# Attention and two feed-forward layers on one core: w_out's rounding copies move to ScalarE, layer 2's weight mixing to GpSimd, and two pieces of work change their place in their engine's order

## The reference, cut to what matters

```python
scores = scale * np.matmul(q, k.transpose(0, 1, 3, 2))
scores = np.where(block_i >= block_j, scores, -1000000000.0)
attn = np.exp(scores - np.max(scores, axis=-1, keepdims=True))
x = (attn / (np.sum(attn, axis=-1, keepdims=True) + 1e-09)) @ v      # heads side by side: (2304, 512)
h = x @ w_in;   g = h * np.clip(h + 3.0, 0.0, 6.0) / 6.0;  x = g @ w_out     # layer 1
h = x @ w_in2;  g = h * np.tanh(log1p(exp(h)));            y = g @ w_out2    # layer 2
```

## Time and profile before

| | us |
|---|---|
| median of 3 runs | 978.65 (973.37 to 980.71) |
| profiled execution | 975.95 |
| its span | 974.0 |
| PE busy in it | 952.0 (98%) |
| DVE, ACT, POOL busy | 746.6, 643.6, 431.3 |
| granted clock, mean | 0.998 |

### The profile page before, as it was taken

How to read it: one execution, slowest core, us unless ns; L and a number is a source line. 1 busy time by engine, 2 the same in 40 slices (tenths; PEclk the granted TensorE clock), 3 DMA queues, 4 the chain that set the end, 5 groups by cost and what they waited for, 6 DMA issues and landing times.

```text
span 974.0 us, 17754 instructions
## 1 busy us (share of the span) xinstructions
PE 952.0 (98%) x6028; PEld 848.0 (87%) x6028; DVE 746.6 (77%) x1417; ACT 643.6 (66%) x1431; POOL 431.3 (44%) x410
## 2 busy tenths in 40 slices
PE   8999999999999999999899999999999999999998
PEld 7898888999887888888788988998998988988896
DVE  7898898774868686789788787777887777777654
ACT  7999999754544445454445557777777777776663
POOL 7899779665837596776867670000000000000000
PEclk9999999999999999999999999999999999999999
DMA  7988898657698978788786546555655654565255
GB/s 217 270 240 243 258 273 234 173 153 238 220 291 291 290 256 252 234 294 252 269 275 212 209 170 217 176 202 195 215 197 184 231 210 155 182 248 187 90 193 194
DMA packets 84601, 216.42 MB, mean 222 GB/s; under 512 B 10144, under 2 KB 16928, under 8 KB 84512
## 3 DMA queue, kind: packets, MB, share of 16 engines
q1 hardware_dynamic: 84368, 215.01, 67.6%
q10 hardware_dynamic: 144, 0.29, 0.1%
HBM read 162.07 MB, written 39.92 MB: 207 GB/s over the span
## 4 chain that ended last, share of the span: by engine, by line
PE 67%; DVE 7%; DMA 6%; SPq 4%; POOL 3%; issue 2%; ACT 1%; ACTq 0%; DVEq 0%; POOLq 0%
PE psum L1021 32%; PE psum L904 10%; PE psum L906 10%; PE psum L905 10%; DMA ext_d<-ext_made 3%; PE psum L849 2%; PE psum L828 2%; DVE ebuf L1624 1%; PE psum L808 1%; POOL osplit L1885 1%; SPq L646 1%; DVE glo L1630 1%; PE psum L809 1%; SPq L648 1%; DVE ext_made L1530 1%
## 5 line engine op out<-in xcount | busy, mean ns | idle before, releaser
L1021 PE MATMUL psum<-ghi,osplit 128*128 128x512 f32 (+1 forms) x640 | 216.7, 372 | 2.1 <-POOL osplit L1885 2.1
L904 PE MATMUL psum<-xhi,whi 128*128 128x256 f32 (+1 forms) x640 | 188.0, 294 | 5.1 <-ACT snap L1242 2.5
L906 PE MATMUL psum<-xhi,wlo 128*128 128x256 f32 (+1 forms) x640 | 187.2, 293 | 0.0
L905 PE MATMUL psum<-xlo,whi 128*128 128x256 f32 (+1 forms) x640 | 187.0, 292 | 0.0
L1021 PE MATMUL psum<-osplit,ghi 128*128 128x512 f32 x576 | 180.7, 395 | 1.3 <-DVE glo L1630 1.3
L1630 DVE SCALAR_TENSOR_TENSOR glo<-ebuf,ghi 128x512 fp32r<-128x512 f32 x144 | 126.5, 878 | 22.9 <-ACT ghi L1290 14.8
L904 PEld LDWEIGHTS psum<-xhi,whi 128*128 128x128 f32 x640 | 121.1, 189 | 19.0 <-ACT snap L1242 4.4
L1290 ACT ACTIVATE ghi<-ebuf 128x512 fp32r<-128x512 f32 x144 | 90.4, 628 | 66.9 <-DVE ebuf L1624 46.2
L1021 PEld LDWEIGHTS psum<-ghi,osplit 128*128 128x128 f32 x640 | 118.5, 190 | 18.4 <-issue 2.7
L1885 POOL TENSOR_TENSOR osplit<-oraw,osplit 128x512 fp32r<-128x512 f32 x80 | 117.2, 1468 | 38.1 <-ACT osplit L1209 34.0
L905 PEld LDWEIGHTS psum<-xlo,whi 128*128 128x128 f32 x640 | 121.2, 189 | 10.5
(11 more groups left out here) (120 smaller groups left out, 2147.4 us busy)
## 6 DMA issues: line engine op xcount, KB each, us to landing
ext<-ext_d SPq DMA_DIRECT2D x56, 768.0 KB, 4.4
osplit<-o_d SPq DMA_DIRECT2D x80, 512.0 KB, 5.3
oraw<-in_w_out SPq DMA_DIRECT2D x80, 256.0 KB, 5.8
wraw<-in_w_in SPq DMA_DIRECT2D x26, 512.0 KB, 6.0
ext_d<-ext_made SPq DMA_DIRECT2D x32, 384.0 KB, 6.2
attn_t<-ostage SPq DMA_DIRECT2D x32, 288.0 KB, 3.7
qkin<-in_qk SPq DMA_DIRECT2D x30, 288.0 KB, 3.7
kparts<-kparts SPq DMA_DIRECT2D x30, 288.0 KB, 4.2
```

The source lines that it names most:

```text
L904: pe.matmul(dst, hi, xh, start=(start and cc == 0), stop=False, skip_group_check=True)
L905: pe.matmul(dst, hi, xl, start=False, stop=False, skip_group_check=True)
L906: last = pe.matmul(dst, lo, xh, start=False, stop=(stop and cc == 1), skip_group_check=True)
L1021: last = pe.matmul(bank(Y_BANK + c, n), stat, mov, start=(first and m == 0), stop=(final and m == 2), skip_group_check=True)
```

## The change

Four edits, all in layer 1's steps:

1. The high halves of w_out's tiles 32 to 79 are made by ACT (split_o_hi in relu_period) and no longer by POOL.
2. The three subtractions of layer 2's extra jobs (steps 19 to 26) are made by POOL (mix_late, with the new semaphore late_mixed), after the step's first low half of w_out, and no longer by DVE.
3. On DVE, extra_jobs and ahead_os of a layer 1 step stand behind the step's two relu products and the first low half of g, no longer before them.
4. On POOL, in step 0, mix_x(1, 1) stands behind the low half of the step's second w_out tile.

```diff
-ACT_OS = TILE0[FIRST_STEP[2]]
 SPLIT_OS = TILE0[LAYER]
...
-MIXED = [sum(3 if e else 1 for _, _, _, e in JOBS[NEARLY:m]) for m in range(len(JOBS) + 1)]
+MIXED = [sum(0 if layer == 1 and e else 3 if e else 1 for layer, _, _, e in JOBS[NEARLY:m])
+         for m in range(len(JOBS) + 1)]
...
             def split_ext_hi(m):
                 layer, p, _, _ = JOBS[m]
-                act.wait_ge(w_mixed, MIXED[m + 1])
+                if layer == 0:
+                    act.wait_ge(w_mixed, MIXED[m + 1])
+                else:
+                    act.wait_ge(late_mixed, 3 * (p + 1))
...
             def first_os(s, k):
 
-                todo = [i for i in splits_at(s) if i < ACT_OS]
+                todo = [i for i in splits_at(s) if i < SPLIT_OS]
...
             def mixing_jobs(s):
                 for m in jobs_at(s)[0:1]:
-                    mix_w(m)
+                    if JOBS[m][0] == 0 or JOBS[m][2]:
+                        mix_w(m)
...
-                extra_jobs(s - 1)
-                ahead_os(s - 1)
                 relu6_times_h(s + 1, 0)
                 relu6_times_h(s + 1, 1)
                 split_g_lo(s + 1, 0)
+                extra_jobs(s - 1)
+                ahead_os(s - 1)
                 mixing_jobs(s)
...
+            def mix_late(m):
+
+                p, raw = JOBS[m][1], wraw[m % 2]
+                a11, a12, a22, a21 = (raw[:, k * A_COLS:(k + 1) * A_COLS] for k in range(4))
+                pool.wait_ge(w_loaded[m % 2], w_level(m))
+                nc.gpsimd.tensor_tensor(a21, a11, a21, ALU.subtract).then_inc(late_mixed, 1)
+                pool.wait_ge(late_mixed, 3 * p + 1)
+                nc.gpsimd.tensor_tensor(a22, a22, a21, ALU.subtract).then_inc(late_mixed, 1)
+                pool.wait_ge(late_mixed, 3 * p + 2)
+                nc.gpsimd.tensor_tensor(a12, a12, a22, ALU.subtract).then_inc(late_mixed, 1)
...
             def split_o(i):
                 o, raw = osplit[i % OS2], oraw[i % OR]
-                if i < FIRST_OS or i >= ACT_OS:
+                if i < FIRST_OS:
...
                 if s == 0:
                     add_x(1, 3)
                     scale_x(1, 3)
-                    mix_x(1, 1)
+                for m in jobs_at(s):
+                    if JOBS[m][0] == 1 and JOBS[m][3]:
+                        mix_late(m)
                 next_x(s, 0)
                 for i in todo[1:2]:
                     split_o(i)
+                if s == 0:
+                    mix_x(1, 1)
                 next_x(s, 1)
```

More of the change, by code:

```diff
@@ L368, in build @@
         w_mixed = sem("w_mixed")
+        late_mixed = sem("late_mixed")
         w_hi = sem("w_hi")
@@ L1881, in split_o @@
                     nc.gpsimd.tensor_copy(o[:, 0:D], raw[:, :]).then_inc(o_hi, 1)
-                    pool.wait_ge(o_hi, i + 1 if i < FIRST_OS else i + 1 - (ACT_OS - FIRST_OS))
+                    pool.wait_ge(o_hi, i + 1)
                 else:
```

## The result

The changed kernel takes 981.23 us (median of 17 runs, 979.46 to 985.83), the kernel before in the same rounds 975.7 (17 runs, 972.48 to 981.07): ratio 1.0068, 95% interval 1.0054 to 1.0082. That is inside the forecast range, but on the other side of the forecast: about 6 us slower, not 1 us faster. The profiled execution took 979.46 us, its span 977.4 us against 974.0; granted clock 0.998 in both.

What follows compares the result with a forecast made beforehand. PE was taken as full from 600 us, with about 14 us reachable in its earlier waits and slow clock. Terms -1.1 - 1.7 - 1.4 - 0.3 - 1.0 + 2.8 + 1.7 = -1.0 us: 975.95 to 975.0, range 963 to 985.

Steps and rivals of the forecast that it cites:

- DVE's order: Moving extra_jobs and ahead_os later on DVE: -1.4 and -0.3 us of PE waits, +3.2 us on block 4's x load.
- The -1.4 at step 10: PE's 1.46 us wait at 317.56 for DVE's relu product, behind the jobs, would go: -1.4 us.
- Steps 0 and 1: Moving mix_x(1, 1) behind a split gains 1.1 us net; the half clock after the wait goes, another 1.7 us.
- Step 17: POOL's chain for block 3 loses five casts, so PE's 1.04 us wait at 401.80 goes: -1.0 us.
- Step 12: PE's wait at 341.98 for ACT's copy goes with DVE's new order: -0.3 us.
- Block 4's chain: x loads and POOL work needed by step 26 take 93.6 us from step 18 against 90.8: PE starts later by 2.8.
- the first rival: POOL is fast enough in steps 18 to 26, nearly all waits go: -11 us, 965 us; chance 0.22.
- The clock: PE's wait of 3 to 4 us before step 26 brings the half clock: +1.7 us.
- The ring (2): Moved DVE job, w_out's loads and ACT hold each other up, 18 us at 7.5 us landing: 988 us; chance 0.10.
- the sign that the prediction named for it: From step 11 on PE would wait for ACT while ACT waits for oraw.

Runs made afterwards that it cites:

- edit 1 with mixing in four steps: Kernel before, with w_out's high halves (tiles 32 to 79) on ACT and POOL mixing layer 2 only in steps 19, 22, 23, 26: ratio 0.9976.
- the jobs between the products: extra_jobs and ahead_os put between DVE's first and second relu product, in several kernels; against the changed kernel's ratio 1.0068, the changed kernel with this: 0.9982.

## Why the prediction was wrong

**The step that failed** is "DVE's order". It saw that SP's queue waits for the moved job and priced the later x load for block 4 only. That price was right: x went out 5.4 us into step 18 (5.6 forecast).

```profile
406.60 0.61 SPq L647 DMA_DIRECT2D xst<-attn_t  x1
```

But the same queue carries block 2's x and w_out's tiles in steps 3 to 10, and there the chain had almost no cover either: before, its last split ended 42.6 us after step 6's start, at 314.29, and PE's first matmul on it came 0.2 us later, without a wait; now the split ends after 45.5.

```profile
314.52 0.29 PE L904 MATMUL psum<-xhi,whi 128*128 128x256 f32 x1
```

Step 9 grew by 2.84 us, 2.58 of it the wait for this split, and the sum had nothing for it; of the changes that were not forecast it is the largest. The place of the jobs behind the second product was read from the order of the list. When that product can run in the new order was not followed (in step 8 it waits 6.63 us, in part for a store in the very queue that the job holds up), although the prediction's own rows for step 18 showed the job 3.5 us late. The -1.4 at step 10 failed too: DVE came 1.30 us late again (1.46 before), 12.13 us for the step. This step varies between executions of the same work: edit 1 alone and edit 1 with mixing in four steps are one program up to step 19 and took 12.49 and 10.89 us; with the jobs between the products it was 10.57 in three kernels and 12.17 in a fourth.

**Steps 0 and 1.** They gained 1.67 us of the 2.8 forecast (1.1 and 1.7), and not by edit 4. In the kernel with edit 1 alone, whose program is the same as before up to step 11, they take 25.1 us. The row answering to the first of the earlier trace rows:

```profile
213.16 0.36 PE L1020 MATMUL psum<-ghi,osplit 128*128 128x256 f32 x1 [1.16 <-POOL osplit L1884]
```

Its wait is 1.16 us, not 2.10, and the clock stays 1.00. Of the twelve profiled kernels without edit 4 (before included) ten take 24.7 to 25.5 us there and two 27.4; the seven with it take 25.1 to 26.1. So before's profile showed an unlucky execution, and I took its 2.10 us and its half clock for the kernel's own; edit 4 alone measures 1.0003. The forecast had no wait left for tile 4 and one of 1.0 us for tile 5. Measured are 1.03 for tile 4, whose low half POOL could start only at 209.39, when ACT's high half was there, and which took 1.80 us, and 0.37 for tile 5: the sum of the two is near, the places are not.

**Step 17**: -1.34 (1.0 forecast), right. **Step 12**: -0.56 (0.3), right.

**Block 4's chain**: right in sum, 94.59 from step 18 to 26 (94.3 forecast: 2.8 on 91.55), and by the places named: ACT held by POOL's mixes in steps 21 and 25 (waits of 1.40 and 0.8), the x split before step 26. Its parts were not right, so that the sum came out is luck. SP's weights load in step 22, then the rows that answer to the earlier trace rows:

```profile
451.06 0.33 SPq L586 DMA_DIRECT2D wraw<-in_w_in  x1
...
417.70 1.30 POOL L1851 TENSOR_TENSOR xst<-xst 128x512 f32<-128x512 f32 x1 [0.65 <-DMA xst<-r_d]
...
445.33 3.18 POOL L1888 TENSOR_TENSOR xlo<-xst,xhi 128x512 fp32r<-128x512 f32 x2
...
464.91 1.29 POOL L1851 TENSOR_TENSOR xst<-xst 128x512 f32<-128x512 f32 x1 [3.55 <-DMA xst<-r_d]
...
491.26 3.11 POOL L1888 TENSOR_TENSOR xlo<-xst,xhi 128x512 fp32r<-128x512 f32 x2
```

What ended last runs through the load of the second half. It went out at 453.00, 51.8 us after step 18's start, 47.5 before: in step 22 too SP stood for the moved job (its weights load comes 6.2 us into the step, 1.2 before), and the forecast had charged that to step 18 alone. From the issue to the first add it took 11.9 us, 14.5 before, which I had not counted; from there to the last split 29.5, 27.4 before. That is 4.4 - 2.6 + 2.0 = 3.8 us later, where 4.2 was forecast.

First add to last split took 30.8 and 29.5 us in the two halves, before 28.3 and 27.4: 4.6 more, where my terms gave about 2. The four mixes cost 13.2 us (10.8 forecast), the two waits for ACT's high half 3.0 (2.2), the ten casts that left gave back 10.0 (8.9), and the other operations, the same in both kernels, took 1.6 us less: the lighter contention on POOL came, at 1.6 of the 2.2 forecast. The groups between 401 and 496, then two groups of the kernel before (400 to 494) that go with the earlier trace rows:

```profile
L1829 POOL TENSOR_TENSOR wraw<-wraw 128x256 f32<-128x256 f32 x7 | 8.8, 1264 | 0.0
L1831 POOL TENSOR_TENSOR wraw<-wraw 128x256 f32<-128x256 f32 x7 | 8.4, 1194 | 0.6
L1833 POOL TENSOR_TENSOR wraw<-wraw 128x256 f32<-128x256 f32 x7 | 5.2, 739 | 0.5
L1635 DVE SCALAR_TENSOR_TENSOR glo<-ebuf,ghi 128x512 fp32r<-128x512 f32 x17 | 21.1, 1239 | 7.7 <-ACT ghi L1294 7.5
L1534 DVE TENSOR_TENSOR ext_made<-wraw,ext_made 128x768 fp32r<-128x768 f32 x7 | 12.1, 1727 | 0.0
```

```profile
L1517 DVE TENSOR_TENSOR wraw<-wraw 128x256 f32<-128x256 f32 x7 | 5.8, 823 | 0.2
L1515 DVE TENSOR_TENSOR wraw<-wraw 128x256 f32<-128x256 f32 x7 | 5.1, 726 | 0.2
```

Three subtractions are 3.2 us on POOL. On DVE they were 2.4 (865, 726 and 823 ns; the prediction took the dearest for all three), so the 21 of this stretch were 17.0 us there, and DVE's busy time fell by 9.9 and not by 20. Its other work got longer: g's low half takes 1239 ns, 1170 before, and the low half of the mixed weights 1727, 1212 before, 3.6 us in seven; the rest is one low half of g and three products more in a longer stretch. With edit 2 alone the two take 1093 and 1449 ns, so the longer times are not that edit's alone, and how the edits share them was not separated. This is what speaks against the first rival: the Trainium skill ("GPSIMD Engine Reference", 8. Key points) names vector instructions with two SBUF inputs among those that collide with GpSimd. Here the subtraction is then a GpSimd instruction beside DVE's other two-input ones, and DVE's rows show no relief. The same section puts elementwise work on DVE at about twice GpSimd's speed; the rows have 805 ns there (the mean of the three) and 1066 here (the mean of 1264, 1194 and 739), 1.3 times as long, both beside a busy neighbour.

**The clock** behind step 26: +1.04 (1.7 forecast), right; 0.69 over the 5 us behind the wait.

**Step 33**, +0.76, was not foreseen. It is in every kernel with edit 1 (11.27 to 11.30 us) and in none without (10.42 to 10.69): POOL now waits there for ACT's high half (3.40 us at 571.09), which in ACT's list stands behind copies of h (the last one begins at 570.00), and block 5's last x split ends at 580.5, PE's first matmul on it at 580.61.

**Rivals.** The ring (2) did not come at its price of 18 us, and PE never waits for w_out's halves in steps 11 to 25. But the sign that the prediction named for it is there once, in step 24: PE waits 2.56 us for ACT's hbuf behind ACT's 2.08 us for oraw. What the rival had not seen is that such a ring closes through the stores of the mixed weights too, as in step 8 above. With the jobs between the products ACT's waits for oraw from 195 to 620 fall from 17.7 to 6.9 us. That POOL is fast enough (1) fell by the 4.2 us wait.

Sum of the measured terms: -0.56 that lie ahead of step 0, -1.67, +2.84, -0.15, -0.56, -1.34, +3.04, +1.04, +0.76 = +3.4 us, which is the difference of the spans. The medians differ by 5.5: the changed kernel's profiled execution is its fastest of 17, before's is near its median. Which of the terms is larger in a typical execution stays open.

## What to carry to other kernels

When a job that others wait for is moved behind an instruction, ask the trace how long that instruction waits, and charge the delay to everything in the queue of whoever waits for the job, not to one transfer. Such a job belongs into the idle place in front of a waiting instruction: here two calls, two lines higher, were worth 0.9%. Then ask whether what the instruction waits for is itself held up by the job, through another engine or a queue; if so, the delay feeds itself. And work given to a helper engine is free only where that engine has no work on the path behind it: with mixing in all eight steps edit 2 cost 0.3 to 0.6% in four pairs of kernels that differ by it (two of them by edit 4 as well), with mixing in 19, 22, 23 and 26 alone nothing that can be seen.

## What the runs showed of the hardware

The clock does not follow the length of the last wait alone. With edit 3 alone PE waited 2.47 us at 316.10 and the next 2.8 us ran at 0.50; in the changed kernel it waited 2.58 us at the same matmul and they ran at 1.00. The windows of the two:

```profile
316.20:319.00 2.80, 2.80 (x9) 2.00 (x9) 2.00 (x4) 2.64 (x5) 0.11 (x1) 0.50 0.55 213
```

```profile
315.10:317.90 2.80, 1.59 (x9) 1.12 (x9) 2.00 (x4) 2.62 (x5) 0.09 (x1) 1.00 0.59 229
```

In the second PE waited another 1.30 us for DVE inside the window, so the half clock of the first cost nothing that shows there: both have nine matmuls in 2.8 us, and step 10 took 11.52 and 12.13 us. The waits of 4.19, 4.57 and 4.4 us before step 26 (changed kernel, edit 2 alone, changed kernel with the jobs between the products) were each followed by slow matmuls: step 26 took 11.54, 11.53 and 12.51 us, 10.50 without such a wait. "TensorE: Matmul & The Clock Gate" of the Trainium skill (Part 1) says that the number of slow matmuls differs from run to run of the same kernel. Steps 0 and 1 above agree: one program up to there, 25.1 us at a clock of 1.00 and 27.4 with 3.4 us at 0.50, where 0.9 us of the difference is a longer wait (2.10 and 1.16 us).
